# GpSimd's work in attention steps 1 to 7 put in the order of steps 8 and up

## The reference

```
q_d = q.reshape(B, H, Sd, factor, D).mean(axis=3)      # k_d, v_d likewise
out_up = np.repeat(softmax(scale * q_d @ k_d.T) @ v_d, factor, axis=2)
mask = abs(pos[:, None] - pos[None, :]) < factor
out_local = softmax(where(mask, scale * q @ k.T, -1e9)) @ v
attn_out = out_up + out_local
```

## Time and profile before

| | us |
|---|---|
| median of 3 runs | 873.81 (873.68 to 875.22) |
| the profiled execution | 875.68 |
| its span in the trace | 873.9 |

### The profile page before, as it was taken

How to read it: one execution, slowest core, us unless ns; L and a number is a source line. 1 busy time by engine, 2 the same in 40 slices (tenths; PEclk the granted TensorE clock), 3 DMA queues, 4 the chain that set the end, 5 groups by cost and what they waited for, 6 DMA issues and landing times.

```text
span 873.9 us, 16199 instructions
## 1 busy us (share of the span) xinstructions
PE 858.0 (98%) x5879; PEld 736.7 (84%) x5879; DVE 538.5 (62%) x782; ACT 505.4 (58%) x910; POOL 202.8 (23%) x279
## 2 busy tenths in 40 slices
PE   8999999999999999999999999999999999999997
PEld 5788887788888888888888988998998998998996
DVE  6777877999999999999985543233233223224222
ACT  4778886889988899888974442222222223223222
POOL 8667864821010041520010002002002002001000
PEclk9999999999999999999999999999999999999999
DMA  9677676378477457431010002002002002000000
GB/s 236 199 232 233 208 228 243 104 268 291 162 264 277 164 189 241 112 88 50 26 61 1 1 1 74 0 1 72 0 0 72 0 0 71 1 0 37 1 0 37
DMA packets 44867, 92.66 MB, mean 106 GB/s; under 512 B 4617, under 2 KB 23929, under 8 KB 40705
## 3 DMA queue, kind: packets, MB, share of 16 engines
q1 hardware_dynamic: 34752, 43.95, 17.0%
q0 software_dynamic: 9872, 47.53, 15.3%
q10 hardware_dynamic: 176, 0.31, 0.1%
HBM read 72.97 MB, written 18.81 MB: 105 GB/s over the span
## 4 chain that ended last, share of the span: by engine, by line
PE 88%; POOL 5%; DVE 2%; issue 2%; ACT 1%; DMA 1%; DVEq 0%; SPq 0%; POOLq 0%; ACTq 0%
PE banks L1044 75%; PE banks L1106 2%; PE banks L962 1%; PE banks L1051 1%; PE banks L940 1%; POOL pin L586 1%; PE banks L904 1%; PE banks L1025 1%; PE banks L851 1%; PE banks L859 1%; PE banks L1126 1%; DVE elo L1763 1%; POOL xs L612 1%; PE banks L916 1%; POOL vpool L594 1%
## 5 line engine op out<-in xcount | busy, mean ns | idle before, releaser
L1763 DVE TENSOR_TENSOR elo<-wslot,ehi 128x1024 fp32r<-128x1024 f32 x196 | 237.1, 1227 | 19.1 <-ACT ehi L1354 13.2
L1354 ACT ACTIVATE ehi<-wslot 128x1024 fp32r (+1 forms) x196 | 205.8, 1059 | 19.5 <-PE banks L1044 18.3
L1857 DVE SCALAR_TENSOR_TENSOR fg<-fraw 128x384 f32<-128x384 f32 x96 | 53.5, 558 | 212.2 <-ACT fraw L1472 203.0
L1472 ACT ACTIVATE fraw<-banks 128x384 f32<-128x384 f32 x96 | 47.2, 492 | 228.1 <-PE banks L1044 224.0
L1044 PE MATMUL banks<-zhi,winhi 128*128 (+1 forms) x384 | 130.4, 340 | 0.2 <-DVE winlo L1781 0.2
L1044 PE MATMUL banks<-zhi,winlo 128*128 (+1 forms) x384 | 129.3, 337 | 0.0
L1044 PE MATMUL banks<-zlo,winhi 128*128 (+1 forms) x384 | 128.9, 336 | 0.0
L1044 PE MATMUL banks<-wouthi,fhi 128*128 128x512 f32 x288 | 113.1, 393 | 2.9 <-DVE flo L1862 1.8
L1044 PE MATMUL banks<-wouthi,flo 128*128 128x512 f32 x288 | 113.9, 395 | 0.0
L1044 PE MATMUL banks<-woutlo,fhi 128*128 128x512 f32 x288 | 113.7, 395 | 0.0
L804 POOL DMA_INDIRECT out_x<-o_sb,row_tok x15 | 15.0, 1000 | 319.0 <-ACT o_sb L1499 316.0
(11 more groups left out here) (233 smaller groups left out, 1451.7 us busy)
## 6 DMA issues: line engine op xcount, KB each, us to landing
wslot<-in_w POOLq DMA_DIRECT2D x24, 1024.0 KB, 6.7
wslot<-in_w SPq DMA_DIRECT2D x8, 1024.0 KB
xr<-xs SPq DMA_DIRECT2D x25, 272.0 KB
ys<-y_sb SPq DMA_DIRECT2D x25, 256.0 KB, 3.4
qb<-in_qT SPq DMA_DIRECT2D x16, 288.0 KB, 3.4
vq<-in_vtok SPq DMA_DIRECT2D x32, 144.0 KB
kb<-in_kT SPq DMA_DIRECT2D x15, 288.0 KB, 5.0
vwin<-in_vtok SPq DMA_DIRECT2D x16, 245.0 KB
```

What stands on the lines that cost most here:

```text
L1354: act.activation(ehi[:, ring_at(k), :], wslot[:, chunk_cols(offs[dt], matrix, half, c)], ACT.Copy).then_inc(s_ehi, 1)
L1472: act.activation(fraw[:, f % 2, :], banks[:, f % 2, 0:TB], ACT.Copy).then_inc(s_fhev, 1)
L1763: dve.tensor_tensor(elo[:, ring_at(k), :], wslot[:, chunk_cols(offs[dt], matrix, half, c)], ehi[:, ring_at(k), :].bitcast(F32), ALU.subtra ...
L1857: dve.scalar_tensor_tensor(out=fg[:, f % 2, :], in0=fraw[:, f % 2, :], scalar=0.01, in1=fraw[:, f % 2, :], op0=ALU.mult, op1=ALU.max).then ...
```

## The change

GpSimd's loop gets one order for all steps of the attention: `normalise(s-1)`, `pool_v(s-1)`, `pool_qk(s+2)`. The functions themselves stay as they are, as do the other engines' streams.

```diff
-                if 2 <= s <= NPAIR:
+                if 1 <= s <= NPAIR:
                     normalise(s - 1)
-                if s >= 8 and 0 <= s - 1 < NPAIR:
                     pool_v(s - 1)
                 if s + 2 < NPAIR:
                     pool_qk(s + 2)
                 if s == 0:
                     constants_as_floats()
-                if s == 1:
-                    normalise(s - 1)
-                if 0 <= s - 1 and s < 8:
-                    pool_v(s - 1)
```

## The result

| | before | changed |
|---|---|---|
| median | 873.74 us (873.61 to 875.22, 4 runs) | 882.52 us (881.49 to 883.37, 4 runs) |
| profiled execution, its span | 875.68, 873.9 | 881.49, 879.8 |
| granted clock, mean of the span | 0.999 | 0.992 |

The measured ratio is 1.0087, with a 95% interval of 1.0057 to 1.0116; it is not the quotient of the two medians, which is 1.0100. The forecast was 875.4 us in a range of 873.6 to 877.2; the result lies outside, and also 5 us above the 877.5 us that the clock rival of the prediction had named.

What follows compares the result with a forecast made beforehand. TensorE, busy 98% of the span, was taken to bound the kernel, GpSimd deciding only step 3's start. Late start 1.55 plus ports 0.05 gave 1.6 us over the median of 873.81: 875.4 us, range 873.6 to 877.2.

Steps and rivals of the forecast that it cites:

- the clock rival: TensorE's clock falls in the 2.8 us gap before pair 3's scores; 2.07 us more, 877.5 us in all; chance 0.10.
- the start of step 3: Where TensorE starts the scores of pair 3; the one place where GpSimd was taken to decide directly.
- The late start, +1.55 us: Step 1 pools pair 3's queries and keys last, so its scores start at 20.77 instead of 19.22 us.
- Ports shared by VectorE and GpSimd, +0.05 us: VectorE's final sum of pair 0 meets GpSimd's key pooling; between 0 and 0.36 us, taken as 0.05.
- the 0.36 of the bound: Upper end of the port term: one VectorE op, the final sum of pair 0's values, 0.36 us on the path.
- Steps 2 to 7, nothing: Later pooling of queries and keys stays covered (1.6 us in step 2), earlier value pooling gains nothing; 0 us.
- VectorE's wait: 1.24 us at 32.18 for pair 2's pooled values; forecast to go, counted 0 because TensorE had 2.29 us of cover.
- The shift lasts: Everything behind pair 3's scores hangs on that pair, so the whole 1.6 us should reach the end.
- The rival in which it is absorbed: Slack behind the attention, near the first expert's weights, eats the shift; 873.8 us, chance 0.12, absorbed or mostly so.
- the clock term: The sum held no loss from TensorE's clock: it was expected to stay at 1.00 through the gap.

Runs made afterwards that it cites:

- the two kernels meant to start it earlier: Step 1 pools pair 3's queries, scales pair 0, pools keys, then values; steps 2 to 7 new: 874.11 us; or old, plus four step-3 fillers: 874.04 us.
- the kernel before with more fillers: Kernel before with fourteen instead of ten filling matmuls in step 2 and four in step 3: 873.98 us, one run of twelve low.

## Why the prediction was wrong

- **What bounds the kernel.** Right as to the place: all of the loss comes from step 1. That the start of step 3 sets the time is shown for a later start; the two kernels meant to start it earlier were no faster.
- **The late start, +1.55 us.** The mechanism was right to the order of events and nearly to the tenth (20.77 forecast, 20.74 and 20.89 seen), but the term was mis-sized, since its other end was not typical. In the first trace GpSimd waited 0.73 us before the queries of pair 3, for a load of keys that took 5.1 us, and I read 19.22 as the old start. In the second profile that wait is gone (13.56), TensorE's gap of 1.66 us is 1.00, and the old start is 18.56. The term is 2.2 us. The medians of the old order near 874.0 and the 876.0 to 876.3 of the new one with its clock up (one run unchanged, two kernels with fillers in the gap) say the same.
- **Ports shared by VectorE and GpSimd, +0.05 us.** Small, as taken, and far from the 0.36 of the bound: the keys' first pooling took 0.73 instead of 0.67 us (at 19.51 in the changed kernel, while VectorE's final sum ran from 19.29 to 19.71), and VectorE's addition took 0.17 us at 18.93, without a wait.
- **Steps 2 to 7, nothing.** Right, shown alone: 0.9995. VectorE's wait went and nobody gained, as forecast.
- **The shift lasts.** Right: 2.2 us at every mark to the end, with steps 7.21 us apart (36.31, 43.52) where the clock stayed up. The rival in which it is absorbed fell.
- **The clock.** Here the prediction failed. The rival that was given one chance in ten happened in 11 of 12 runs of the changed kernel. The step that failed is the clock term, which the sum put at nothing: against a fall I set only that a gap of 1.66 us had left the next transposes at 1.07 us, and I had no row for a gap of 2.8. What the runs showed in its place is a fall in most runs that costs 6.9 us (882.9 less the 876.0 of the run that kept its clock), three times the late start. Its price in the rival was wrong too: 2.07 us, from ten fillers at the lower level, took the spell to be as short as those, but it lasted 13.5 us in the first profile and cost 5.4 us there. Four fillers in step 3 took 3.3 us off the median (879.2). My idea behind them, that TensorE's waits for ScalarE keep the clock down, fits that but isn't shown: the first profile has one such wait in the spell, and 10 us of busy TensorE behind it before the clock rises.

The rule of the Trainium skill (TensorE: Matmul & The Clock Gate, "Part 1: The HAM clock gate"), that the clock goes to half after idleness, was the one that spoke against this change, and the traces agree with it in kind: 1.00 before the gap and 0.50 behind it in the changed kernel's first profile, and a low mean in 15 of the 18 runs with this gap and no added filler. It deserved the larger chance.

What stays open: why one gap of 2.83 us brings the clock down and the next does not (3 of those 18 runs kept it), what keeps it down for 10 us of busy work, and what made the load late in the profile of the kernel before with more fillers.

## What to carry to other kernels

When an edit moves a wait on TensorE, work out the gap that it leaves there and compare it with the longest gap that the trace shows at full clock. A gap beyond that is a case of its own, and here a likely one; its price goes with the length of the spell behind it, 3.4 to 17 us in these traces, and not with the gap. Matmuls that nothing reads, put into the gap, took that price away here (six or twelve of them, none of 17 runs low). And before a term is measured against one trace, look whether the row it starts from waited for a load: take that wait out to see the usual run.
